# Three edits in an attention and two-layer FFN kernel: a two-tile add, an earlier product on GpSimd, fewer products ahead of the first scores

## What is computed

```python
q_pool = q.reshape(B, H, S // 2, 2, D).mean(axis=3)
scores = scale * np.matmul(q_pool, k.transpose(0, 1, 3, 2))
scores = scores - np.max(scores, axis=-1, keepdims=True)
attn = np.exp(scores)
attn = attn / (np.sum(attn, axis=-1, keepdims=True) + 1e-09)
out = np.matmul(attn, v)
# x: the heads side by side, 1152 tokens x 512
h = x @ w_in;  x = (h * np.tanh(np.log1p(np.exp(h)))) @ w_out       # first layer (mish)
h = x @ w_in2; y = np.where(h > 0, h, np.exp(h) - 1) @ w_out2        # second layer (elu)
```

## Time and profile before

| | us |
|---|---|
| median of 3 runs | 679.12 |
| lowest and highest | 677.97, 679.26 |
| the profiled execution | 678.26 |
| its span, first to last instruction | 676.5 |
| TensorE busy in it | 657.4 |

### The profile page before, as it was taken

One profiled execution on the slowest core, in us unless ns is written; L12 is line 12 of the kernel. 1 busy time (PEld: TensorE's weight loads), 2 busy tenths in 40 slices (PEclk: granted clock), 3 DMA queues, 4 the chain that ended last, 5 costly groups with the idle time before them and its releaser, 6 DMA issues.

```text
span 676.5 us, 12456 instructions
## 1 busy us (share of the span) xinstructions
PE 657.4 (97%) x4034; PEld 641.5 (95%) x4034; DVE 412.7 (61%) x708; ACT 391.1 (58%) x733; POOL 419.6 (62%) x384
## 2 busy tenths in 40 slices
PE   7899999999999999999999999999999999999998
PEld 6899899999999999999999999999999999999998
DVE  7678878787888872687776665777553232223222
ACT  5688888888888878555565555555633322222221
POOL 5587697979797866587776775777554422222221
PEclk9999999999999999999999999999999999999999
DMA  6556566655656421121110001221222010001001
GB/s 201 163 157 182 160 185 179 174 172 172 188 160 187 131 69 45 46 81 64 63 31 0 0 0 47 64 62 63 63 79 74 21 47 0 0 0 47 1 1 47
DMA packets 35856, 57.92 MB, mean 86 GB/s; under 512 B 7568, under 2 KB 13024, under 8 KB 35808
## 3 DMA queue, kind: packets, MB, share of 16 engines
q1 hardware_dynamic: 35488, 57.02, 28.7%
q10 hardware_dynamic: 320, 0.30, 0.2%
HBM read 33.29 MB, written 2.40 MB: 53 GB/s over the span
## 4 chain that ended last, share of the span: by engine, by line
PE 76%; DVE 9%; ACT 6%; POOL 4%; issue 3%; DMA 1%; ACTq 0%; POOLq 0%; DVEq 0%
PE py L584 9%; PE py L585 9%; PE py L586 9%; PE pH L569 8%; PE pH L570 8%; PE pH L571 8%; PE ps L501 4%; PE po L517 4%; PE ps L502 4%; PE pm L487 4%; PE po L518 4%; PE po L519 4%; DVE pl L857 3%; ACT ps L671 2%; ACT ph L669 2%
## 5 line engine op out<-in xcount | busy, mean ns | idle before, releaser
L1086 POOL TENSOR_TENSOR gl<-fg,gh 128x384 fp32r<-128x384 f32 x96 | 98.0, 1021 | 134.8 <-ACT gh L763 133.2
L837 DVE TENSOR_REDUCE part_max<-pm 128x1 f32<-128x384 f32 x225 | 117.9, 550 | 31.2 <-PE pm L487 28.5
L584 PE MATMUL py<-gh,wout_h 128*128 128x384 f32 x384 | 129.1, 336 | 1.9 <-DVE xl L942 1.2
L1029 POOL TENSOR_TENSOR pl<-p,ph 128x576 fp32r<-128x576 f32 x72 | 105.7, 1472 | 39.1 <-ACT p L675 38.0
L585 PE MATMUL py<-gl,wout_h 128*128 128x384 f32 x384 | 128.3, 334 | 0.0
L586 PE MATMUL py<-gh,wout_l 128*128 128x384 f32 x384 | 128.3, 334 | 0.0
L571 PE MATMUL pH<-xh,win_l 128*128 (+1 forms) x384 | 128.3, 334 | 0.0
L570 PE MATMUL pH<-xl,win_h 128*128 (+1 forms) x384 | 128.3, 334 | 0.0
L569 PE MATMUL pH<-xh,win_h 128*128 (+1 forms) x384 | 128.3, 334 | 0.0
L669 ACT ACTIVATE ph<-ps 128x576 fp32r<-128x576 f32 x144 | 93.8, 651 | 40.4 <-PE ps L502 37.4
L921 DVE RECIPROCAL fi<-fp 128x192 f32<-128x192 f32 x48 | 64.9, 1352 | 52.4 <-POOL fp L1094 52.4
(11 more groups left out here) (79 smaller groups left out, 1359.8 us busy)
## 6 DMA issues: line engine op xcount, KB each, us to landing
kh<-k_hi SPq DMA_DIRECT2D x60, 144.0 KB, 3.1
w_raw<-w_in SPq DMA_DIRECT2D x32, 256.0 KB, 2.7
w_raw<-w_out SPq DMA_DIRECT2D x32, 256.0 KB, 2.6
q_raw<-qT SPq DMA_DIRECT2D x16, 288.0 KB, 3.0
k_pack<-kP SPq DMA_DIRECT2D x16, 288.0 KB, 3.3
v_raw<-v SPq DMA_DIRECT2D x16, 288.0 KB, 3.3
kl<-k_pack SPq DMA_DIRECT2D x32, 144.0 KB, 2.4
q<-q SPq DMA_DIRECT2D x16, 144.0 KB, 2.5
```

Source lines behind the costliest of these rows:

```text
L584: pe.matmul(out, hi, gh[:, f % 4, :], start=(f == 0), stop=False)
L837: dve.tensor_reduce(part_max[:, par, j:j + 1], pm[:, at % 2, 0:MC], AX.X, ALU.max).then_inc(m_read, 1)
```

## The change

It makes three edits, and adds one tile.

1. `WARM_ROW` goes from 16 to 28, `WARM_SCORES` from 6 to 2 and `EARLY_CHUNKS` from (3, 2) to (2, 3): twelve more unread products behind the maximum of head 0, four fewer ahead of the first scores, and one of the products of head 1 passes from in front of the first two score tiles to behind them.
2. `invert` adds a tile that holds 1e-9 (`least_sum`, set once at the start of VectorE's program, with a semaphore of its own) in place of a constant.
3. In GpSimd's unit step of the first layer `multiply_d(u)` comes ahead of `finish_mish(u-1)`.

```diff
-WARM_FIRST, WARM_ROW, WARM_SCORES = 20, 16, 6
+WARM_FIRST, WARM_ROW, WARM_SCORES = 20, 28, 2
-EARLY_CHUNKS = (3, 2)
+EARLY_CHUNKS = (2, 3)
...
+            least_sum = sa("least_sum", [P, FEW])
...
             def invert(p):
 
+                if p == 0:
+                    dve.wait_ge(preset_least, 1)
                 dve.wait_ge(sums_in[0], 16 * (p + 1))
                 dve.wait_ge(sums_in[1], 16 * (p + 1))
-                dve.tensor_scalar(sum_few[:, :], sum_few[:, :], 1e-9, None, ALU.add).then_inc(sum_kept, 1)
+                dve.tensor_tensor(sum_few[:, :], sum_few[:, :], least_sum[:, :], ALU.add).then_inc(sum_kept, 1)
...
             dve.memset(row_max[:, :, :].bitcast(F32), 0.0).then_inc(preset_row, 1)
+            dve.memset(least_sum[:, :], 1e-9).then_inc(preset_least, 1)
...
                 if layer == 0:
-                    first = isinstance(u, int) and u == 0
-                    if not first:
+                    multiply_d(f, u)
+                    if not (isinstance(u, int) and u == 0):
                         finish_mish((f + 3) % 4, u - 1)
-                    multiply_d(f, u)
-                    if not first:
                         split_g((f + 3) % 4, u - 1)
```

More of the change, by code:

```diff
@@ L150, in build @@
         first_filled, first_read = sem("first_filled"), sem("first_read")
-        warm_set, first_half = sem("warm_set"), sem("first_half")
+        warm_set, first_half, preset_least = sem("warm_set"), sem("first_half"), sem("preset_least")
         s_filled, s_read = sem("s_filled"), sem("s_read")
```

## The result

| | before | after |
|---|---|---|
| median, us | 678.93 | 687.73 |
| lowest and highest | 677.97, 679.26 | 686.17, 690.21 |
| the profiled execution | 678.26 | 688.81 |
| its span | 676.5 | 686.9 |

The account below looks back on a forecast made before the run. TensorE, 97% busy, was taken as the bound, with the elementwise chain pacing tile 0. Order +8.2, start -0.4 and add -0.2 sum to +7.6 us, giving 686.7 us, range 682.5 to 691.0.

Parts of the forecast that it names:

- The new cycle: First layer: the reorder closes a one-unit cycle through ScalarE (gh to fd) and GpSimd (fp, fg), above TensorE's 4.16 us.
- shorter form: Cycle of gh, weight rounding, sigmoid, square, fd, fp, fg and the next gh, without a low part: 4.33 us a unit.
- GpSimd's own order with a low part: Odd units: GpSimd's sequence of fg, gl, low_w, fp and fg takes 4.60 us.
- the mean: Average of units with and without GpSimd's low part: 4.47 us a unit, against 4.32 in tile 0 and TensorE's 4.16.
- Tiles 0 and 2: First-layer tiles with weight work: the reorder costs +4.1 us in tile 0 and +3.6 us in tile 2.
- The sum of the order: GpSimd reorder over the first layer's three tiles: +8.2 us together, bounds +3.8 and +13.8.
- Tile 1: First layer without weight work: cycle of 3.81 us loses nothing in the steady part; +0.5 us at its start (0 to 1.2).
- The start: TensorE's first scores come 2.2 us sooner, but only 0.4 us is left behind the wait for v_raw: -0.4 us.
- it lands when it did: The v_raw DMA, queued on SP behind others that don't wait for the scores, was claimed to land at an unchanged time, 26.37.
- the rival at 0.2: TensorE idles about 2 us near 28 us, then the clock halves, losing 1.7 us: 688.4 us; chance 0.2.
- The add: VectorE's add of 1e-9 in invert, from a tile instead of a constant: -0.2 us, bounds 0 to -1.
- The comparison with the reciprocal's 215 ns: If VectorE's new add took as long as the same-size reciprocal (0.215 us), VectorE would be spared 3 us.

Follow-up runs that it names:

- x13_order_low_dve: New GpSimd order, and the first layer's odd low parts moved from GpSimd to VectorE, against the kernel before: 680.84 us, +1.9 (1.0030).
- x5_order_ahead: New GpSimd order, and ScalarE's sigmoid, square and fd made one unit ahead, against the kernel before: 678.79 us, -0.2 (0.9993).
- x1_order: Only GpSimd's unit step reordered, multiply_d ahead of finish_mish, against the kernel before: 686.90 us, +7.9 (1.0118).
- x14_tile1: GpSimd's new order in tile 1 of the first layer only, against the kernel before: 679.38 us, +0.5 (1.0006).
- x2_start: Only the three start numbers changed (WARM_ROW, WARM_SCORES, EARLY_CHUNKS), against the kernel before: 679.60 us, +0.6 (1.0007).
- x15_row28: Only WARM_ROW raised to 28, against the kernel before: 678.91 us, 0.0 (1.0007).
- x6_start_v: Start edits, and the load of v for head 1 issued earlier on SP, against the kernel before: 676.39 us, -2.6 (0.9961).

## Why the prediction was right, point by point

**The new cycle** is shown. Its shorter form was put at 4.33 us and is 4.30 (in the changed kernel and, alone, in `x13_order_low_dve`); GpSimd's own order with a low part was put at 4.60 and is 4.65; the mean, put at 4.47, is 4.475. Two terms of the longer one were off and cancelled in part: end of `fg` to `gl` is 0.64 (0.79), `gl` to `low_w` 1.20 (0.98). Edits on either side of it, in `x5_order_ahead` and `x13_order_low_dve`, take away what the account says they should in tile 2. Tile 0 is less regular: its pace is uneven in every kernel, and a mean per unit gave its sum. One detail was wrong: `fp` follows `fd` directly in odd units, and stands behind `low_w` in even ones, since the low part of an odd unit comes at the end of its step; I had it the other way round. No number hung on it.

**Tiles 0 and 2** were put at +4.1 and +3.6; they are +4.3 and +3.6 in the changed kernel, +4.0 and +3.6 in `x1_order`. The sum of the order, +8.2, is +7.9.

**Tile 1** was mis-sized: +0.5 in the forecast, -0.1 in three kernels (changed, `x1_order`, `x14_tile1`). The loss that I looked for is there (unit 16 to 17 takes 4.68 us, 4.29 before), but unit 15 to 16 gives more back (4.24, 4.84 before), where the old order had its own wait. These stretches begin at unit 15. `x14_tile1`, where unit 14 to 15 can be told from tile 0's own loss, has +0.3 over units 14 to 17, so that the forecast's loss is real and half as large.

**The end of the layer** wasn't in the sum: unit 47 to 48 takes 5.32 instead of 5.02, +0.3.

**The start** was put at -0.4, with "it lands when it did" as its ground. (The rows give less: `pl` sooner by 28.44 - 28.17 = 0.27 us.) That step failed: the DMA's queue order was unchanged, and `v_raw` still landed 1.55 us later. Alone, the edit costs 0.6 in the median: it gives 0.3 in the group whose clock holds, and costs 1.3 in the other. So, by the mean clock, the rival at 0.2 came true in about half of the executions. That its price of 1.7 us is close to the distance of the groups (1.6 in `x2_start`, 2.1 in `x15_row28`) is partly luck, since in the profiled executions the distance holds the later landing too, which the rival hadn't. The ground that I gave against it, that nothing says that this idle time lies as the other did, was no ground: there were over 2 us of idle time in my own list of what should appear. The Trainium skill (TensorE: Matmul & The Clock Gate, HAM oscillation) describes waits between groups of products that bring the clock down. The traces agree in part: 0.50 behind idle times of 3.18, 2.81 and 1.87 us, and 1.00 in `x6_start_v`, where these waits are gone, but also 1.00 behind the 2.42 us of `x1_order`. The page has it for longer waits than the shortest of these, so it didn't settle the rival as the prediction took it to; here the measurement decides.

**The add** was put at -0.2 and is 0.0. It takes 157 to 1341 ns in the changed kernel:

```profile
L867 DVE TENSOR_TENSOR sum_few<-sum_few,least_sum x8: 157/498/1341, 68.0 to 287.8; 128x9 f32<-128x9 f32 x8
```

The 157 ns are those of the add at 287.75, the only one of the 24 in three kernels that meets no GpSimd instruction. The others are as long as the GpSimd instruction beside them goes on, in the old form and in the new. The comparison with the reciprocal's 215 ns was the wrong one. By the rule that the prediction cites for a VectorE instruction with two SBUF inputs (SBUF — State Buffer, Who interferes with whom, in the Trainium skill) the term is 0, and the runs agree with that.

**The medians.** The forecast of 686.7 was 1.0 below 687.73. The order (7.9) and the start (0.6) give 8.5 of the measured 8.8 us; the profiled execution, at a low clock, shows 10.4. That the forecast came as near as 1.0 us rests on the order's sum; the start was off by 1.0 in the median and by 3.0 in the profiled execution.

## What to carry to other kernels

When an instruction is moved ahead of another on one engine, write down the new cycle that this closes, with every engine in it, before counting what the old one saves: here both engines were 60% busy, and the cycle through them was still longer than TensorE's 4.16 us. The cure was not an earlier place for the product but a unit's worth of distance on both engines, so that each takes up work that was finished before (a reserve of 3.16 us in tile 0). And a gain at the start of a queue is worth only what the next landing lets through; move that load first.

## What the runs showed of the hardware

**An issue of a DMA can take three times as long.** `v_raw` took 0.58 us to issue in the kernel before and in `x15_row28`, 2.05 in the changed one and 1.84 in `x2_start`. In `x6_start_v` another one did, `k_pack` at 24.63 with 1.31 us. In the changed kernel, between 23 and 27 us, the DMA view has one packet of another kind (queue, kind: packets, MB, share of 16 engines):

```profile
q8 instruction: 1, 0.02, 2.3%
```

By its kind I take it for a fetch of instructions. It starts at 23.5 us in the changed kernel and in `x2_start`, at 24.3 in `x6_start_v`, and at 26.5 in the kernel before, when SyncE issues nothing. So in three kernels the slow issue and the fetch fall together, and it would fit that TensorE, 2 us ahead, asks for its instructions 2 to 3 us sooner. In `x15_row28`, where the load landed late with an issue of normal length, the fetch starts at 25.4: behind the issue, but 2.6 us ahead of the landing. In the kernel before it starts as the load lands (26.37), and in `x1_order` 0.5 us ahead of it (26.5 and 26.96). So in all three executions with the late landing the fetch came while the load was under way. That it is the cause is argued, not shown: no run moved the fetch by itself.

**The half clock doesn't follow from the idle time alone.** Ahead of the products at 16 us, 1.87 us of idle time in the kernel before were followed by 3.41 us at 0.50, and 2.42 us in `x1_order`, with the same program up to there, were not. Near 30 us the profiled executions have it behind 3.18, 2.81 and 1.87 us. By their mean clock, 7 of 12 executions of `x2_start` and 5 of 12 of `x15_row28` had a drop somewhere and the others had none, and the groups are 1.6 and 2.1 us apart. How much of this is the clock can only be estimated from the profiled ones: the seventh tile's scores are 1.1 to 1.3 us late ahead of the half clock, and unit 0 of the first layer 2.0 to 2.5 us late (282.11, 282.54 and 282.62 against 280.14), which leaves 0.9 to 1.2 us. A kernel that lies at that edge has two times, and its median says which is more frequent, not what an edit costs.

**A small add on VectorE waits for GpSimd.** The 128x9 add takes 0.16 us when GpSimd does nothing, and up to 1.35 us when it starts just behind the start of a GpSimd instruction of 1.4 us. Both forms do, the one with a constant and the one with a tile, while the reciprocal of the same tile takes 215 ns every time.
